# Chunks of 384, 384, 384, 512 and 640 tokens in place of 384, 512, 384, 512 and 512, with the order of all five engines planned anew

## What is computed

```python
scores = scale * np.matmul(q, k.transpose(0, 1, 3, 2))
thresh = np.max(scores, axis=-1, keepdims=True) - tau
scores = np.where(scores >= thresh, scores, -1000000000.0)
attn = softmax(scores)                 # sum + 1e-09 below
x = attn_out.transpose(0, 2, 1, 3).reshape(B * S, H * D)      # 2304 x 512
p = domain_probs / (domain_probs.sum(-1, keepdims=True) + 1e-09)
for e in range(E):
    h = np.maximum(x @ w1[e], 0.0)
    out += p[:, e:e + 1] * (h @ w2[e])
```

## Time and profile before

| | |
|---|---|
| time, median of 3 runs | 1090.0 us (1089.19 to 1090.68) |
| the profiled execution, its own time | 1088.7 us |
| its span, first to last instruction | 1086.7 us |
| PE busy in the span | 1061.0 us (98%) |
| DVE, ACT, POOL busy | 674.6, 562.2, 629.0 us |
| granted TensorE clock | 1.00 throughout |

### The profile page before, as it was taken

How to read it: one execution, slowest core, us unless ns; L and a number is a source line. 1 busy time by engine, 2 the same in 40 slices (tenths; PEclk the granted TensorE clock), 3 DMA queues, 4 the chain that set the end, 5 groups by cost and what they waited for, 6 DMA issues and landing times.

```text
span 1086.7 us, 17018 instructions
## 1 busy us (share of the span) xinstructions
PE 1061.0 (98%) x5752; PEld 931.5 (86%) x5752; DVE 674.6 (62%) x1505; ACT 562.2 (52%) x990; POOL 629.0 (58%) x659
## 2 busy tenths in 40 slices
PE   5899999999999999999999999999999999999998
PEld 5789899899888888888899999988888888888887
DVE  6988788787887788777777878752122133343331
ACT  6776566666766647566475656644233232242330
POOL 6756576767886748667486867656444342232220
PEclk9999999999999999999999999999999999999999
DMA  6534344445544424223333433333333244233311
GB/s 163 155 111 123 87 123 133 131 128 156 148 148 120 137 57 121 92 85 115 103 124 111 127 115 116 90 100 123 94 110 88 72 123 136 87 107 97 107 58 39
DMA packets 96788, 121.08 MB, mean 111 GB/s; under 512 B 41152, under 2 KB 45248, under 8 KB 96704
## 3 DMA queue, kind: packets, MB, share of 16 engines
q1 hardware_dynamic: 96400, 119.68, 37.0%
q10 hardware_dynamic: 304, 0.33, 0.1%
HBM read 115.25 MB, written 4.72 MB: 110 GB/s over the span
## 4 chain that ended last, share of the span: by engine, by line
PE 92%; DVE 4%; issue 1%; ACT 1%; POOL 1%; DMA 1%; SPq 0%; ACTq 0%; DVEq 0%
PE e_ps L863 12%; PE e_ps L865 12%; PE e_ps L864 12%; PE e_ps L848 12%; PE e_ps L850 12%; PE e_ps L849 12%; PE t_ps L794 6%; PE s_ps L782 3%; PE x_ps L821 3%; PE s_ps L783 3%; PE x_ps L823 3%; PE x_ps L806 1%; DVE p L1002 1%; DVE small L991 1%; DVE q_hl L972 0%
## 5 line engine op out<-in xcount | busy, mean ns | idle before, releaser
L760 POOL TENSOR_TENSOR w_lo<-stage,w_hi 128x512 fp32r<-128x512 f32 x272 | 355.8, 1319 | 275.6 <-ACT w_hi L950 275.3
L950 ACT ACTIVATE w_hi<-stage 128x512 fp32r<-128x512 f32 x320 | 194.1, 625 | 177.3 <-PE e_ps L865 120.6
L848 PE MATMUL e_ps<-x_hi,w_hi 128*128 128x512 f32 (+1 forms) x640 | 241.3, 377 | 0.2 <-DVE h_lo L1042 0.2
L850 PE MATMUL e_ps<-x_hi,w_lo 128*128 128x512 f32 (+1 forms) x640 | 236.2, 369 | 0.0
L849 PE MATMUL e_ps<-x_lo,w_hi 128*128 128x512 f32 (+1 forms) x640 | 235.8, 368 | 0.0
L863 PE MATMUL e_ps<-w_hi,h_hi 128*128 128x512 f32 x576 | 229.8, 399 | 0.0
L865 PE MATMUL e_ps<-w_hi,h_lo 128*128 128x512 f32 x576 | 225.2, 391 | 0.0
L864 PE MATMUL e_ps<-w_lo,h_hi 128*128 128x512 f32 x576 | 224.8, 390 | 0.0
L1042 DVE SCALAR_TENSOR_TENSOR h_lo<-e_ps,h_hi 128x512 fp32r<-128x512 f32 (+1 forms) x160 | 101.8, 636 | 127.1 <-ACT h_hi L940 125.1
L940 ACT ACTIVATE h_hi<-e_ps 128x512 fp32r<-128x512 f32 (+1 forms) x160 | 88.6, 554 | 118.0 <-PE e_ps L850 117.2
L904 ACT ACTIVATE p<-s_ps,small 128x576 f32<-128x576 f32 x132 | 97.4, 738 | 73.2 <-DVE small L991 72.7
(11 more groups left out here) (64 smaller groups left out, 1465.0 us busy)
## 6 DMA issues: line engine op xcount, KB each, us to landing
stage<-w SPq DMA_DIRECT2D x320, 256.0 KB, 2.9
k_raw<-kT SPq DMA_DIRECT2D x94, 144.0 KB, 2.8
v_raw<-v SPq DMA_DIRECT2D x40, 128.0 KB, 2.2
out<-acc SPq DMA_DIRECT2D x18, 256.0 KB, 2.0
q_raw<-qT SPq DMA_DIRECT2D x32, 144.0 KB, 2.9
q_raw<-qT SPq DMA_DIRECT2D x16, 96.0 KB, 2.6
v_raw<-v SPq DMA_DIRECT2D x80, 16.0 KB, 2.1
q_raw<-qT SPq DMA_DIRECT2D x16, 80.0 KB, 2.4
```

What stands on the lines that cost most here:

```text
L760: gp.tensor_tensor(w_lo[:, m % RING, :], stage[:, m % STAGES, :], w_hi[:, m % RING, :], ALU.subtract).then_inc(s_wl, 1)
L848: mm(ps[:, 0:n], w_hi[:, piece, tile], x_hi[:, k, cols], start=k == 0, stop=False)
L850: op = mm(ps[:, 0:n], w_lo[:, piece, tile], x_hi[:, k, cols], start=False, stop=k == KT - 1)
L950: run(w_hi[:, m % RING, :], stage[:, m % STAGES, :], copy).then_inc(s_wh, 1)
```

## The change

The last chunk is 640 tokens wide, so its `up` groups are cut in two halves of 320 columns, and chunk 1 has 384 tokens instead of 512. Units beside the chunks: 24 beside chunk 0, 24 beside chunk 1, 36 beside chunk 2, 36 beside chunk 3. The number of units, of attention's passes over a head (6 visits of 4 head pairs) and of passes over the weights (5) is as before. The hidden tiles grow from 512 to 640 columns and the `x` ring shrinks from 1408 to 1152; the fifth `acc` tile lies in `x_sum`, which attention no longer needs by then. The planner's tables have other numbers, and its slack now has a value for each kind of step that another engine releases, transfers among them.

```diff
-X_COLS = 1408
-X_FIRST = 128
+X_COLS = 1152
+X_FIRST = 0
 CHUNKS = tuple((n, (X_FIRST + first) % X_COLS, first)
-               for n, first in ((384, 0), (512, 384), (384, 896), (512, 1280), (512, 1792)))
-WIDEST = 512
+               for n, first in ((384, 0), (384, 384), (384, 768), (512, 1152), (640, 1664)))
+WIDEST = 640
...
-          (1, 0, 384, 192, (0, 384, 0, 384)), (1, 1, 0, 320, (0, 0, 0, 0)),
-          (2, 1, 320, 256, (0, 512, 256, 0)), (2, 2, 0, 576, (0, 384, 0, 384)),
-          (3, 3, 0, 576, (0, 384, 0, 384)))
+          (1, 0, 384, 192, (0, 384, 0, 384)), (1, 1, 0, 192, (0, 384, 0, 384)),
+          (2, 1, 192, 384, (0, 0, 0, 0)),
+          (3, 2, 0, 576, (0, 384, 0, 384)),
+          (4, 3, 0, 576, (0, 384, 0, 384)))
...
-PLAN = dict(first=3.59, period=2.76, experts=17.92, end=13.35, weights=35.63, weight=8.82, prob=19.0)
+PLAN = dict(first=3.47, period=2.42, experts=18.25, end=13.72, weights=35.74, weight=8.68, prob=16.67)
...
-SLACK = 0.4
+
+SLACK = dict(s=0.31, tr=0.4, pv=1.15, pv32=0.77, up=0.36, down=-0.01, q_load=0.5, k_load=0.49, v32_load=2.1,
+             v_load=1.47, w_load=3.68, store=2.8, p_out=-1.38, p_in=5.51)
...
-            if awaits[s] == 0 and step[1:] != ("slack",) and ENGINE[s[0]] == "PE" and ENGINE[step[0]] != "PE":
+            slack = SLACK.get(s[0])
+            if awaits[s] == 0 and step[1:] != ("slack",) and slack and ENGINE[step[0]] != ENGINE[s[0]]:
...
-        acc = sb("acc", [P, WIDEST // P, D])
+        acc = sb("acc", [P, WIDEST // P - 1, D])
...
+        def acc_tile(j):
+
+            return acc[:, j, :] if j < WIDEST // P - 1 else x_sum[:, 0:D]
```

More of the change, by code:

```diff
@@ L206, in ups_through @@
     return (UPS_TO[t - 1] if t else 0) + (f + 1) * len(col_parts(CHUNKS[t // E][0]))
[L212 to L217, removed]
-PLAN = dict(first=3.59, period=2.76, experts=17.92, end=13.35, weights=35.63, weight=8.82, prob=19.0)
+ALONE = dict(load=-2.53, q_hi=6.22, q_lo=15.17, k_hi=4.15, k_lo=-5.57, v_hi=9.15, v_lo=-7.93, max=9.03, thr=13.9,
+             exp=5.12, mask=11.77, eps=15.71, rec=6.52, norm=24.71, tr=-2.83, phi=17.75, plo=18.15, pv=22.7,
+             xo=24.84, xs=7.69, x_hi=-7.24, x_lo=5.07)
+AMONG = dict(load=-6.91, q_hi=2.06, q_lo=5.4, k_hi=-7.36, k_lo=-8.63, v_hi=-1.69, v_lo=10.31, max=-6.48, thr=-3.72,
+             exp=7.36, mask=0.01, eps=-13.84, rec=2.04, norm=-0.5, tr=9.74, phi=8.77, plo=-1.91, pv=13.78, xo=2.23,
+             xs=10.1, x_hi=7.92, x_lo=3.04)
+PLAN = dict(first=3.47, period=2.42, experts=18.25, end=13.72, weights=35.74, weight=8.68, prob=16.67)
 def halves_of(u):
@@ L495, in release @@
             awaits[s] -= 1
[L496 removed]
+            slack = SLACK.get(s[0])
+            if awaits[s] == 0 and step[1:] != ("slack",) and slack and ENGINE[step[0]] != ENGINE[s[0]]:
                 awaits[s] = 1
                 then[s, "slack"] = [s]
[L499 removed]
+                landing.append((now + slack, len(order), (s, "slack")))
             elif awaits[s] == 0:
@@ L713, in _ @@
                     first = CHUNKS[g.c][2] + g.j * P
-                    sp.dma_start(out[first:first + P, :], acc[:, g.j, :]).then_inc(s_out, 16)
+                    sp.dma_start(out[first:first + P, :], acc_tile(g.j)).then_inc(s_out, 16)
             sp.wait_ge(s_out, 16 * TT)
@@ L1054, in _ @@
                             dve.wait_ge(s_out, CHUNKS[g.c][2] // P * 16)
-                        ve.tensor_scalar(acc[:, g.j, :], e_ps[:, g.bank, :], weight, None, ALU.mult
+                        ve.tensor_scalar(acc_tile(g.j), e_ps[:, g.bank, :], weight, None, ALU.mult
                                          ).then_inc(s_acc, 1)
@@ L1058, in _ @@
                         dve.wait_ge(s_acc, g.index + 1 - CHUNKS[g.c][0] // P)
-                        ve.scalar_tensor_tensor(out=acc[:, g.j, :], in0=e_ps[:, g.bank, :], scalar=weight,
-                                                in1=acc[:, g.j, :], op0=ALU.mult, op1=ALU.add).then_inc(s_acc, 1)
+                        ve.scalar_tensor_tensor(out=acc_tile(g.j), in0=e_ps[:, g.bank, :], scalar=weight,
+                                                in1=acc_tile(g.j), op0=ALU.mult, op1=ALU.add).then_inc(s_acc, 1)
 def kernel(q, k, v, tau, moe_domain_probs, moe_w1, moe_w2):
```

## The result

The change makes the kernel slower by 0.3%: 1094.59 us (median of 15 runs, 1093.36 to 1095.80) against 1090.68 us for the kernel before, run beside it (15 runs, 1089.19 to 1094.77). The ratio is 1.0029, with a 95% interval of 1.0021 to 1.0037. The forecast was 1094.4. Term 5 and the offset between profile and median were wrong all the same, and term 4 was too small; the rest of this text is mostly about these three.

A forecast was written before the change was run, and what follows sets the result against it. PE, 98% busy, was taken as the bound. Terms of 5.4 + 1.3 + 1.4 - 1.3 - 2.4 = +4.4 us on the profiled 1088.7 gave 1093.1, and 1.3 of offset made it 1094.4, range 1089.5 to 1099.0.

The forecast's parts named there:

- Term 5: PE's waits in the middle: 3.4 us of early `pv` and `s` shrink to 1.0 under the new order, -2.4 us.
- the offset between profile and median: The profiled execution of before lies 1.3 us below the runs' median, so 1.3 is added to the forecast.
- term 4: First stage: new order saves DVE's wait for unit 24's exponential and part of a `q_lo`, -1.3 us.
- term 1: Matmuls of `up`: same columns in 384 more matmuls, 13.5 ns fixed cost each, +5.4 us.
- Term 2: Matmuls of `pv`: other widths of the parts in each visit, +1.3 us.
- Term 3: Half groups in the last chunk: `h_lo` late by 0.34 us at four starts of experts, +1.4 us.
- some 2.4 was named as a sign: PE's waits from the first `up` to the end should be about 2.4 us, those on `h_lo` included.
- The order pays for the matmuls: Rival: savings in the first stage and middle offset the extra matmuls, no change, 1090.6 us; chance 0.18.
- A new wait: Rival: weight pieces come late at the end of `up` in chunks 0 to 2, 1099.4 us; chance 0.10.
- Extra matmuls are free: Rival: the extra matmuls of `up` cost nothing of their own, 1089.0 us; chance 0.03.

The follow-up runs named there:

- b_cut256: The kernel before with its 512-column `up` groups cut into two of 256, 1152 more matmuls; 1119.29 us, ratio 1.0264.
- a_lo_pool: The changed kernel with all `w_lo` pieces of the last chunk on POOL, none on DVE; 1093.17 us, ratio 1.0015 to the kernel before.
- b_newplan: The kernel before with its own chunks and visits, but the planner's tables and slacks of the change; 1095.97 us, ratio 1.0044.
- b_splice: The kernel before with only each engine's first-stage steps in the new plan's order, all later steps in the old order; 1085.79 us, ratio 0.9952.
- b_qfirst: The kernel before with the q transfer of head 3 put ahead of the k transfer of head 4 in SP's queue; 1088.56 us, ratio 0.9979.
- a_oldplan: The changed kernel's chunks, visits and tiles with the planner's tables and single slack of before; 1111.49 us, ratio 1.0181 to the kernel before.
- a_klfirst: The changed kernel with the k transfer of head 4 put ahead of the q transfer of head 3; 1098.42 us, ratio 1.0068 to the kernel before.
- a_noxfer: The changed kernel with the values for transfers and stores taken out of its planner's slack; 1106.85 us, ratio 1.0142 to the kernel before.

## Why the prediction was right, and where only in its sum

**Terms 1 and 2, +5.4 and +1.3: right, and term 1 shown.** The matmuls by their distances grew by 6.7 us. b_cut256 measured the part of a cut by itself, 13.5 ns a matmul in a chunk without waits. Term 2 has no run of its own and rests on the distances at 192 to 384 columns. By the figure of the Trainium skill (TensorE: Matmul & The Clock Gate, section "Wait — 56ns, not 53.3ns?") of 2.5 ns that chunk would have grown by an estimated 1.0 us; it grew by 5.2. The measurement decides.

**Term 3, +1.4: right, and shown.** Chunk 4 took 223.05 us, 1.34 more than its matmuls; a_lo_pool took the two `w_lo` from ahead of `h_lo` and had the 1.4 us back. Each `h_lo` was late by 0.28 us and not 0.34, and the 0.10 at the next start was in no term.

**Term 4, -1.3: the mechanism right, the size off.** It was -2.3. The gain is where it was named, ahead of the mask of unit 25: the 0.9 for the exponential of unit 24 came, and the `q_lo` moved behind the mask gave 0.5 for the 0.35 counted. What was undersized is the rest of the new order, which the forecast couldn't read and put at nothing: the maximum of unit 23, done earlier, gave some 0.8. The same order of the first stage was worth 2.7 us in a_lo_pool, 3.6 in b_newplan and 3.9 in b_splice, so -2.3 is the least of four executions.

**Term 5, -2.4: wrong.** It was +0.3. The step that failed is "PE's 3.4 us are a `pv` put too soon [...] and an `s` too soon", read as all that could be had. I took PE's list of waits for a full account. By the distances of starts, chunks 0 to 3 held 11.85 us of excess before, and 12.12 after. The named long waits did go; others came in at the masks and transposes of other units. That the list came out at 2.5 us, where some 2.4 was named as a sign, was no support: it holds nothing of the 1.4 us on `h_lo` in chunk 4, and 2.5 of other waits where 1.0 was allowed. Nor do the new slack and tables save waits by themselves: with them on the old chunks (b_newplan) PE waited more.

**The offset, +1.3: wrong for the changed kernel.** I added to both kernels what separated the median of before from its profile. Between the two profiled executions lie +5.9 us and not +4.4 (term 5 was 2.7 more than forecast, term 4 1.0 less). Between the medians lie +3.9: the profiled execution of before lies 2.0 us below its median, and that of the changed kernel on it. b_qfirst shows that one swap in SP's queue is enough to take that loss away from the kernel before. These two errors cancelled: that the time was right within 0.2 us was luck, and the account of it was not right.

**The rivals.** "The order pays for the matmuls" has its core in b_splice: there the order paid 3 to 5 us, all of it in the first stage; in this kernel it paid 2.3 there, too little for the matmuls. "A new wait" for weight pieces didn't come: no wait on `w_lo` or on a transfer is in PE's list. "Extra matmuls are free" is refuted by b_cut256.

**Open.** Which of the new order's moves carries the first stage's gain in the faster executions isn't parted further. Nor is it shown what makes the small fixed part of the excess at each change from one kind of matmul to another, and why both orders keep some 6 us of late starts. That most executions of the kernel before lose their 2 us by a late `q` and a fall of the clock behind the gap at 31 us is argued from b_qfirst's runs and from two kernels with the same order; no profiled execution of that kernel caught it.

## What to carry to other kernels

Cutting a matmul in two costs its fixed part on the engine that is the bound, so a layout that needs cuts has to win that elsewhere; measure the part as the distance of starts at two widths. Sum those distances by stage and compare them with the stage's length, because the list of waits of an engine whose ends are modelled leaves out the small waits. An order fitted to one layout is worth little on another, but its stretches can be tested one by one, as b_splice does, and before a forecast the profiled execution is to be held against the median: if they differ by more than the scatter, something happens in most executions that the profile doesn't show.

## What the runs showed of the hardware

- Gaps of 1.9 to 3.4 us on PE in the middle of work were followed by a lower granted clock over the next 4 us: 0.65 after 1.88 (a_oldplan), 0.62 after 3.16 (b_cut256), 0.62 around 1.87 and 0.67 after 3.39 (a_klfirst). In a_klfirst matmuls of 288 columns then started 0.24 us apart instead of 0.132. The length of one gap doesn't decide it: behind 1.84 us in b_splice and 1.75 in the changed kernel (31.08) the clock stayed at 1.00, while in a_noxfer it was 0.60 from 56 to 60 us with gaps of no more than 0.89 (54.48) and 1.00 us (56.21) ahead.
- A transfer of the same size, issued at the same place of the same order, landed after 3.2 us in one execution and after some 4.9 in another (`q_raw`, issued at 26.57 and 26.72; ACT starts on it at 29.79 and 31.59).
- In the changed kernel the first `w_lo` of chunk 4 took 0.69 us on DVE and the second 1.37 (rows above). POOL's timeline has a `w_lo` of its own beside the second, from 867.90 to 869.20 (no run took it away while the second stayed on DVE):

```profile
867.90 1.30 POOL L768 TENSOR_TENSOR w_lo<-stage,w_hi 128x512 fp32r<-128x512 f32 x1 [10.90 <-ACT w_hi L958]
```

- Matmuls of 192 columns start 0.111 us apart and those of 256 0.120, while from 320 to 512 each column costs 0.416 ns.
